# Attention, token mixing and a gated feed-forward in one program: the range is judged from alpha, the first mixed tile sits among the last pairs, and half of the token weights are split in the first batch

## What is computed

```python
# attention, per batch and head: 32 heads, 768 tokens, head width 48
state = alpha[t, :, None] * state + outer(k[t], v[t]);  x[t] = q[t] @ state
# mixing, per batch: x is (768, 384)
theta = x @ w_theta
y = w_tok_r @ (x * cos(theta)) + w_tok_i @ (x * sin(theta))
u = x + y;  u = u + relu(u @ w_ch)
# feed-forward, width 1024, conv over 3 neighbouring tokens
h = relu(u @ w_in);  out = (h * sigmoid(conv(h))) @ w_out
```

## Time and profile before

| | us |
|---|---|
| median of 3 runs | 584.03 |
| lowest, highest | 581.27, 584.75 |
| the profiled execution | 583.93 |
| its span, first to last instruction | 582.2 |

### The profile page before, as it was taken

How to read it: one execution, slowest core, us unless ns; L and a number is a source line. 1 busy time by engine, 2 the same in 40 slices (tenths; PEclk the granted TensorE clock), 3 DMA queues, 4 the chain that set the end, 5 groups by cost and what they waited for, 6 DMA issues and landing times.

```text
span 582.2 us, 11688 instructions
## 1 busy us (share of the span) xinstructions
PE 544.3 (93%) x4026; PEld 521.4 (90%) x4026; DVE 433.7 (74%) x657; ACT 269.9 (46%) x571; POOL 223.0 (38%) x191
## 2 busy tenths in 40 slices
PE   3899999855999999999999998999999999999996
PEld 2777787745999999999999998999999999999996
DVE  6999898715565856584648464789989899998984
ACT  3666566523343443344334454254454545545543
POOL 7777787601241124112411257033323333333332
PEclk9999999977999999999999999999999999999999
DMA  8999999451200210022002201120220202011011
GB/s 186 283 278 275 284 281 277 143 164 43 63 17 26 96 63 14 27 95 63 14 27 78 86 1 41 42 83 9 74 82 0 81 0 81 34 47 42 0 42 41
DMA packets 33909, 52.11 MB, mean 89 GB/s; under 512 B 3536, under 2 KB 23760, under 8 KB 33872
## 3 DMA queue, kind: packets, MB, share of 16 engines
q1 hardware_dynamic: 31472, 48.08, 29.4%
q10 hardware_dynamic: 2400, 3.54, 1.7%
HBM read 37.45 MB, written 14.16 MB: 89 GB/s over the span
## 4 chain that ended last, share of the span: by engine, by line
PE 62%; issue 9%; POOL 3%; DVE 2%; ACT 2%; ACTq 0%; POOLq 0%; DVEq 0%
PE y_bank L1063 24%; PE y_bank L1113 13%; PE theta_bank L1053 7%; PE theta_bank L1101 6%; PE x_bank L1101 6%; PE y_bank L1084 5%; POOL z L831 3%; PE x_bank L1044 1%; POOL mixing_w L824 0%; DVE turns L945 0%; ACT z L864 0%; DVE angle L955 0%; ACT L873 0%; DVE angle L952 0%; DVE x_t L936 0%
## 5 line engine op out<-in xcount | busy, mean ns | idle before, releaser
L1063 PE MATMUL y_bank<-mixing_w,z 128*128 128x384 f32 x864 | 155.9, 337 | 1.9 <-POOL z L810 1.8
L1063 PEld LDWEIGHTS y_bank<-mixing_w,z 128*128 128x128 f32 x864 | 148.9, 188 | 3.2 <-POOL z L810 3.2
L831 POOL TENSOR_TENSOR z<-x_tokens,z 128x384 fp32r<-128x384 f32 x64 | 68.6, 1073 | 146.0 <-ACT z L914 129.1
L1113 PE MATMUL y_bank<-mixing_w,z 128*128 128x384 f32 x576 | 111.3, 337 | 2.7 <-POOL z L831 2.7
L810 POOL TENSOR_TENSOR z<-z_full,z 128x384 fp32r<-128x384 f32 x48 | 49.2, 1047 | 167.3 <-ACT z L864 167.3
L1113 PEld LDWEIGHTS y_bank<-mixing_w,z 128*128 128x128 f32 x576 | 101.7, 188 | 3.6 <-POOL z L831 2.3
L1021 DVE SCALAR_TENSOR_TENSOR z_full<-out_rows,taps,x_rows 128x384 f32<-128x384 f32 x64 | 79.2, 1237 | 2.3
L1101 PE MATMUL theta_bank<-mixing_w,in_w 128*128 128x386 f32 x288 | 55.7, 337 | 0.0
L1101 PE MATMUL x_bank<-mixing_w,in_w 128*128 128x386 f32 x288 | 55.7, 337 | 0.0
L1101 PEld LDWEIGHTS theta_bank<-mixing_w,in_w 128*128 128x128 f32 x288 | 50.9, 188 | 0.0
L1101 PEld LDWEIGHTS x_bank<-mixing_w,in_w 128*128 128x128 f32 x288 | 50.9, 188 | 0.0
(11 more groups left out here) (93 smaller groups left out, 842.9 us busy)
## 6 DMA issues: line engine op xcount, KB each, us to landing
a_in<-in_a_rows SPq DMA_DIRECT2D x32, 146.2 KB, 6.7
k_in<-in_k_rows SPq DMA_DIRECT2D x32, 144.0 KB, 6.3
q_in<-in_q_rows SPq DMA_DIRECT2D x32, 144.0 KB, 7.0
v_in<-in_v_tokens SPq DMA_DIRECT2D x16, 288.0 KB, 6.9
x_scratch<-x_rows SPq DMA_DIRECT2D x32, 144.0 KB, 6.2
x_in<-x_scratch SPq DMA_DIRECT2D x24, 192.0 KB, 2.5
y<-x_all SPq DMA_DIRECT2D x7, 576.0 KB, 3.3
u_scratch<-u_sum ACTq DMA_DIRECT2D x6, 576.0 KB, 3.6
```

What stands on the lines that cost most here:

```text
L831: pool.tensor_tensor(g[k % 4][1][:, :], gated[k % 2], g[k % 4][0][:, :].bitcast(F32), ALU.subtract).then_inc(g_low.sem, 1)
L1063: ins = pe.matmul(y_bank[2 * d + half][:, 0:HALF], z[s % 2][part][zp][:, d * P:(d + 1) * P], mixing_w[part][wp][:, s, half * HALF:(half + ...
L1113: ins = pe.matmul(out_bank[half][t][:, 0:MODEL], g[k % 4][gp][:, t * P:(t + 1) * P], out_w[wp][f], start=f == 0 and i == 0, stop=f == FF_T ...
```

## The change

All stages become one program with one list, `program`, from which each engine takes the places that it fills. Line numbers below this point are those of the new kernel where a diff or a list of it is shown.

- The range is judged from alpha itself: ACT compares each pair's alpha with a least value, 0.625 (`compare`), two steps ahead of the scans. For this `a_in` has four buffers instead of two. In step 0 ACT compares pairs 0, 1 and 2. `magnitudes` goes.
- In step 14 PE and DVE sum the shortfalls (`judge`); then SP, PE and DVE each read `in_range` and branch (`decide`). SP also reads a batch number into a register, by which the last stores of x are aimed. SP then loads the first three x tiles.
- Steps 16 and 17 of the pairs become `pair_tail`, in which the work of tile 0 of batch 0 (turn, theta, angle, sines, product, split) and part of tile 1's stands between that of pairs 14 and 15. The barriers between the programs go.
- Attention takes 7 pieces instead of 14, one every second step: w_theta and the token weights of tiles 0 to 2. The other 7 are loaded and split in batch 0, which is now written out (`load_weight`, in `mix_batch`); batches 1 and 2 are the loop. They use two raw buffers in `out_rows`, and w_out is loaded in batch 3.
- The layout of some buffers changes (`rest_w`, `u_c`), not their sizes per instruction.

```diff
 # step 0 and following of the pairs
-                    act.activation(magnitudes[:, :], before[i % 2][:, :], ACT.Abs, accum_out=sums[:, i:i + 1]).then_inc(measured.sem, 1)
+        for n in range(0 if i == 0 else i + 2, min(i + 3, PAIRS)):
+            do.compare(n)
+        def compare(n):
+            got_a[n % 4].done(act, n // 4)
+            measured.done(act, n - 1)
+            act.activation(shortfall[:, :, :], packed(a_in[n % 4][:, :], 1), ACT.Relu, bias=least[:, 0:1], scale=-1.0,
+                           accum_out=sums[:, n:n + 1]).then_inc(measured.sem, 1)
+        for n in range(2, 4):
+            sp.wait_ge(pads, 5 + n)
+            rows(a_in, a_rows, got_a, n)
...
 # step 14
+            if i == JUDGED_AT:
+                do.judge()
+        if i == JUDGED_AT:
+            do.decide()
+            do.load_first()
+        def judge():
+            dve.wait_ge(all_measured, 1)
+            dve.tensor_reduce(total[:, :], shortfalls, mybir.AxisListType.X, ALU.add).then_inc(judged, 1)
+            dve.wait_ge(judged, 1)
+            dve.tensor_scalar(in_range[:, :], total[:, :], 0.0, None, ALU.is_le).then_inc(judged, 1)
+            dve.tensor_scalar(x_batch[:, :], total[:, :], 0.0, float(LAST), ALU.is_gt, ALU.add).then_inc(judged, 1)
+        def decide():
+            pe.wait_ge(judged, 3)
+            by_state.if_out_of_range(pe, in_range, by_state.path_tensor)
...
 # pieces of weights
+    def piece_of(i):
+        n = i // 2 - 1
+        return n if i % 2 == 0 and 0 <= n < ATTENTION_PIECES else None
+            tile(do.round_z, b, s + 1, last)
+            if isinstance(b, int) and b == 0:
+                do.load_weight(s)
+            if s == 2 and not last:
+                do.spare(b)
+        def refill_piece(n):                      # SP
+            piece_low.done(sp, n - 2)
+            sp.dma_start(raw_of(n), pieces[n].source).then_inc(got_piece[n % 2].sem, 16)
+        def load_weight(s):                       # SP
+            if s == 0:
+                mixed.done(sp, 0)
+            for n in range(ATTENTION_PIECES + 2 * s, min(ATTENTION_PIECES + 2 * s + 2, len(pieces))):
+                refill_piece(n)
+        def load_weight(s):                       # POOL; ACT has the same with high(n)
+            for n in range(ATTENTION_PIECES + 2 * s - 2, min(ATTENTION_PIECES + 2 * s, len(pieces))):
+                if n >= ATTENTION_PIECES:
+                    low(n)
+            if first_batch:                       # PE, mix
+                piece_low.done(pe, 2 + 2 * s)
```

More of the change, by code:

```diff
@@ L28 @@
 TWO_PI_LOW = 2 * np.pi - TWO_PI_HIGH
-IN_RANGE = 2.0 ** 60
 ROUND = 1.5 * 2.0 ** 23
@@ L54, in before @@
         eng.wait_ge(self.sem, (n + (self.lead - back + 1)) * self.per)
[L61 to L83, removed]
+PASSES = ((0, 0), (0, 1), (1, 0))
 CHUNK = P
@@ L458, in attention_by_token @@
-        block = ctx.enter_context(nc.Block())
-        def halves(tile):
-            return tile.rearrange("p (h t) -> p h t", h=2)
+        self.names = "akqv"
+        self.rows = {x: sb(x + "_rows", [P, SEQ]) for x in self.names}
+        self.chosen = sb("chosen", [P, 2 * SLOT])
+        self.heads = sb("heads", [P, 2])
+        self.added, self.states, self.read = (sb(x, [P, SEQ]) for x in ("added", "states", "read"))
+        self.x_pair = sb("x_pair", [2, SEQ])
+        self.got, self.used = tally("got", 16 * 8), tally("used", 1, 1)
@@ new lines, in path_vector, with halves, path @@
+    def path_vector(self, ident, reset):
+        rows, chosen, heads, added, states, read = self.rows, self.chosen, self.heads, self.added, self.states, self.read
+        def halves(tile):
+            return tile.rearrange("p (h t) -> p h t", h=2)
+        def path(dve):
+            self.used.open(dve)
+            self.x_copied.open(dve)
+            for x in self.names:
+                dve.memset(rows[x][:, :], 1.0 if x == "a" else 0.0).then_inc(self.const, 1)
+            dve.memset(heads[:, :], 0.0).then_inc(self.const, 1)
+            dve.wait_ge(self.const, 5)
@@ L531, in path_vector @@
-                    scanned.done(dve, i, 1)
-                    dve.tensor_tensor_scan(states[:, :], rows["a"][:, :], added[:, :], 0.0, ALU.mult, ALU.add).then_inc(scanned.sem, 1)
-                    scanned.done(dve, i, 2)
-                    dve.tensor_tensor(read[:, :], rows["q"][:, :], states[:, :], ALU.mult).then_inc(scanned.sem, 1)
-                    x_made.done(dve, i)
-                    stored.before(dve, i, 1)
-                    dve.tensor_copy(halves(x_pair[:, :]), x_sum[:, :, 0:HALF]).then_inc(x_copied.sem, 1)
@@ new lines, in path @@
+                    self.scanned.done(dve, i, 2)
+                    dve.tensor_tensor(read[:, :], rows["q"][:, :], states[:, :], ALU.mult).then_inc(self.scanned.sem, 1)
+                    self.x_made.done(dve, i)
+                    self.stored.before(dve, i, 1)
+                    dve.tensor_copy(halves(self.x_pair[:, :]), self.x_sum[:, :, 0:HALF]).then_inc(self.x_copied.sem, 1)
+                self.x_copied.done(dve, n * HEAD_DIM + HEAD_DIM - 1)
+                dve.sem_inc(self.used.sem, 1)
@@ new lines, in path, with nothing @@
+            reset(self.const, self.n_const)
+            dve.wait_ge(self.const, self.n_const + 2)
+        return path
+Piece = namedtuple("Piece", "source high low raw_of")
+def nothing(*_):
+    pass
+PLACES = """refill_piece scale_q back by_token inside keep scan_after scale_k spread added high feed compare scan_before low
+refill judge score mask scan_state decide store halve hold turn theta angle sines product round_z load load_first
+load_weight spare prepare mix sums end join front gate split back_ff fetch""".split()
```

1756 lines of the change are left out of this document (899 added, 857 removed).

## The result

| | before | changed |
|---|---|---|
| median (four executions of each, same chip), us | 582.78 | 589.23 |
| lowest, highest | 581.27, 584.75 | 588.44, 590.8 |
| the profiled execution, its span | 583.93, 582.2 | 589.34, 587.2 |
| mean granted clock of the profiled execution | 0.988 | 0.991 |

The ratio is 1.0112, with a 95% interval from 1.0069 to 1.0155: about 6.5 us slower. The prediction was 586.8, with a range from 577 to 594. The sign and the place of the loss were right. One term of 3.8 us was missing, and the others together were 1.7 us too high, most of it in batch 0, which covered nearly half of it.

What follows compares the result with a forecast made beforehand. The prediction took PE to set the pace in attention, with PE busy nearly throughout mixing and half idle in the passage between. Its sum was 583.93 + 4.2 - 0.7 - 13.9 + 13.3 = 586.8 us, range 577 to 594.

Steps and rivals of the forecast that it cites:

- What bounds: In attention PE sets the step at 6.55 us and the DMAs keep up; 13 steps gain 0.7 us.
- Rival (a): In attention the loads set the pace, so 13 steps gain 7.3 us instead of 0.7: 580.2; chance 0.07.
- The start, +4.2: ACT's first copy of turned k waits behind the third pair's alpha comparison, 4.2 us late; bounds 2.5 to 6.
- Rival (c): At the start, alpha lands by 9.5, so the start costs nothing: 582.6; chance 0.10.
- The passage, -13.9: From step 14 to the first mix, 38.5 us become 24.6, a gain of 13.9; bounds 12.4 to 15.4.
- The branch: In the passage, reading the flag and branching costs PE and DVE 1.5 us, between nothing and 3.0.
- Batch 0, +13.3: In mixing's batch 0, `in_rows` queued behind piece 12 stalls DVE: tile 4 11.4 late, tile 5 1.9; bounds 9 to 14.4.
- M: The start of tile 0's mix in batch 0, from which the prediction counts that batch's times in us.
- cast to the end of that split, 6.84: In batch 0, from DVE's cast of `in_rows` to the end of tile 5's split of x: 6.84 us.
- Rival (b): In batch 0, `in_rows` does not hold DVE, 11.4 us less: 575.4, or 573.9 with a free branch; chance 0.15.
- Rival (d): After batch 0's gap the clock stays at half through tile 4's mix, another 6.25: 593.0; chance 0.22, including costlier branches.
- edits at nothing: The comparison outside the start, w_out's load, ACT's rounding, the two-batch loop and the feed-forward cost nothing.

Runs made afterwards that it cites:

- changed + 64: The changed kernel with an unused tile of 64 bytes per partition ahead of `x_tokens`; 588.7 us.
- the last experiment: The kernel with three edits, with POOL's scaling of the last pair's q also waiting for DVE's low part of the first x tile; 574.13 us, ratio 0.9835.
- three edits: The changed kernel with batch 0's spare at tile 4's place, the third alpha comparison in step 1, and 32 unused bytes ahead of `x_tokens`; 574.9 us, ratio 0.9864.

## Why the prediction was right, and where it was not

- **What bounds.** Right. The steps of attention went from 6.63 to 6.55 us, the pace of PE, although landings of alpha over the whole span fell from 6.7 to 4.4 us. Rival (a), with 7.3 us to gain from fewer loads, fell by this.
- **The start, +4.2.** Right in place and size: +4.5, and 3.8 of it came back when the comparison was moved. The copy was forecast for 14.7 and came at 15.02. Rival (c) fell.
- **The passage, -13.9.** Right in sum (-14.2) and wrong in two terms that cancel. From pair 14's turning to the first mix it took 130.97 - 106.87 = 24.1 us, forecast 24.6. The branch, set at 1.5 from bounds of 0 and 3.0, does not show in these 24.1 us at all: it lies ahead of 106.87. That turning starts 6.86 after the one before it (100.01), where a step takes 6.55, and PE's weight loads were idle for 0.29 us ahead of it; so the branch cost 0.3 at most. On DVE it ran under the mask at 105.28, and the state scan behind that follows without a gap. Its lower bound would have been the better choice. The Trainium skill ("Advanced Engine Details and Errata", section "Control Flow Timing") gives a compare-and-branch about 108 ns. No run here shows it alone, since the 0.29 holds the read of the flag too. In its place stood a collision of DVE and POOL over x_t, 1.77 us of waiting PE, where 0.6 had been set for the split. That the sum came out within 0.3 is luck.
- **Batch 0, +13.3.** Right in mechanism, somewhat too large. Issue at M + 29.0 (forecast 29.2), cast at M + 33.7 (33.2), theta of 3.25 us (3.24), tile 4's mix 9.6 late against its own due time (11.4), tile 5 2.6 later still (1.9), 0.75 of it from a mix that began at the lower clock. The term that was too large is "cast to the end of that split, 6.84": the old 6.84 us held a wait for theta that the new order does not have (164.65 to 170.02 now, 5.37), so theta came at M + 39.1 and not at M + 40.0. The loss without the slower products is 12.7 - 0.7 = 12.0.
- **Does L952 wait for POOL?** The operation that was left open (now L990, both inputs in SBUF) took 1.50 us under POOL's pieces and 0.56 without them. It waits. The rule of the Trainium skill quoted in the prediction ("SBUF — State Buffer", section "Who interferes with whom") agrees with the trace.
- **Rival (b)** (faster, `in_rows` does not hold DVE) fell in the changed kernel, and was made true by moving one issue: 7.8 us of span. **Rival (d)** (half clock through tile 4's mix, +6.25) fell: that mix took 7.35 instead of 6.60.
- **What was missing.** "Batches 1 to 3 at 8.14 a tile" and "the feed-forward stays as it is" were wrong: a tile takes 8.27, and this and the feed-forward make +3.8 (0.7, 1.7 and 1.4). The step that failed is "edits at nothing": the prediction took a changed layout for free since it changes no instruction's size. Unused bytes alone do the same to the kernel before: 59.2 us a batch instead of 58.5, and 3.2 us in its median.

Without the slower products the change would have been +1.2 in the span, where +2.9 was forecast; with them it is +5.0. The forecast lies between the two because its errors had opposite signs. The stall was foreseen; that the number came so near is in part luck.

## What to carry to other kernels

When a change puts loads into a queue that must wait for an engine, look at what stands behind them in that queue, and who waits for it with more behind: here one DMA issue, movable at no cost, was worth 7.8 us of span. When work is moved to fill a gap, count the collisions of DVE with POOL that it brings, at the size of POOL's whole instruction. And after any change of buffers compare the durations of an unchanged instruction before and after, in every batch and not in one: a pace that is off by 2% over the whole kernel is not in any wait.

## What the runs showed of the hardware that was not expected

- Where operands lie in SBUF changes TensorE's pace at full clock. With the stationary operands of theta and of the mix (128 x 128, fp32r) 32 bytes past a multiple of 256 in their partition, 36 products took 6.60 us instead of 6.49, in both kernels; at 96 some mixes did, with the same tiles as others that did not, and at 64, 128, 160 and 224 none. Products back took 1.75 instead of 1.72 also at 128. So the residue alone is not the rule, and other residues and sizes were not tried.
- The granted clock can fall after a gap of under 2 us, and need not: mixes behind waits of 1.82 and 1.84 us took 8.08 (changed + 64, and the last experiment), one behind 1.85 took 6.51 (three edits).
- A cast of 1024 elements to fp32r took DVE 0.69 us alone, and 1.35 and 2.16 beside a subtraction on POOL (the one beside the 1.35 ran from 163.46 to 165.90).
